# Last block's third w_in chunk loaded beside the fourth; a rank inside a second layer; the last routing steps reordered

## What is computed

```python
# 1. attention, 2 batches x 8 heads x 576 tokens x 64, keeping the 32 largest scores of a row
scores = q @ k.T / sqrt(64);  attn = softmax(scores where scores >= 32nd largest of the row)
x = (attn @ v)                         # -> 1152 tokens x 512
# 2. dense layer pair with a parametric relu
h = x @ w_in;  g = max(h, 0) + alpha * min(h, 0);  x2 = g @ w_out    # 512 -> 2048 -> 512
# 3. mixture of 8 experts, each token to its best 2
noisy = x2 @ w_gate + log1p(exp(x2 @ w_noise)) * noise
top2 of noisy per token; weights = softmax over those two
out[token] += weight * (relu(x2 @ w1[e]) @ w2[e])     # 512 -> 1024 -> 512
```

## Time and profile before

| what | value |
|---|---|
| median of 3 runs | 728.12 us (727.68 to 728.68) |
| the profiled execution | 731.02 us, of which the span of its instructions is 729.3 us |
| TensorE busy (matmul) | 663.6 us, 91% of the span |
| VectorE (DVE) busy | 528.5 us, 72% |
| ScalarE (ACT) busy | 466.8 us, 64% |
| GpSimd (POOL) busy | 392.9 us, 54% |
| attention of the last block ends | about 424 us |
| first expert item starts on TensorE | 477.08 us |

### The profile page before, as it was taken

One profiled execution on the slowest core, in us unless ns is written; L12 is line 12 of the kernel. 1 busy time (PEld: TensorE's weight loads), 2 busy tenths in 40 slices (PEclk: granted clock), 3 DMA queues, 4 the chain that ended last, 5 costly groups with the idle time before them and its releaser, 6 DMA issues.

```text
span 729.3 us, 13745 instructions
## 1 busy us (share of the span) xinstructions
PE 663.6 (91%) x4688; PEld 563.9 (77%) x4688; DVE 528.5 (72%) x1112; ACT 466.8 (64%) x881; POOL 392.9 (54%) x436
## 2 busy tenths in 40 slices
PE   2467789999989999999999999899999999999993
PEld 2346667887867888888888777688998999989993
DVE  5999999989769989898998352695565555555520
ACT  5788876787887787787777645755354553544511
POOL 3598898788787777677767766220220311302112
PEclk9987989999999999999999999999999999999997
DMA  9879436645418535264563769735935738457222
GB/s 284 357 257 386 153 153 226 237 161 184 189 20 282 184 132 213 92 245 161 194 212 116 276 236 353 240 118 192 291 100 205 223 103 279 122 181 238 72 32 36
DMA packets 39964, 141.01 MB, mean 193 GB/s; under 512 B 11152, under 2 KB 12176, under 8 KB 35856
## 3 DMA queue, kind: packets, MB, share of 16 engines
q1 hardware_dynamic: 35520, 130.25, 49.9%
q0 software_dynamic: 4384, 9.98, 6.3%
HBM read 113.70 MB, written 45.73 MB: 219 GB/s over the span
## 4 chain that ended last, share of the span: by engine, by line
PE 70%; POOL 13%; ACT 6%; issue 4%; DVE 4%; DMA 1%; SPq 0%; POOLq 0%; ACTq 0%; another core or an unknown queue 0%; DVEq 0%
PE bank L1261 11%; PE bank L1079 11%; PE ps_scores L1245 10%; PE bank L1042 7%; PE bank L1245 6%; PE bank L1018 6%; POOL expo L1763 4%; PE bank L1266 4%; PE bank L1047 3%; PE bank L1000 3%; PE ps_scores L969 3%; POOL w_in_parts L1775 2%; POOL k_parts L1720 2%; PE bank L1059 2%; PE bank L1280 1%
## 5 line engine op out<-in xcount | busy, mean ns | idle before, releaser
L441 DVE MAX8 top<-rest 128x8 f32<-128x576 f32 x216 | 152.4, 748 | 0.0
L1923 POOL DMA_INDIRECT out_dram<-ye,xe x24 | 42.8, 1785 | 190.0 <-ACT ye L1661 164.6
L1763 POOL TENSOR_TENSOR expo<-scores,expo 128x576 f32<-128x576 f32 x72 | 103.8, 1442 | 60.8 <-ACT scores L1354 60.6
L453 DVE MATCH_REPLACE8 rest<-top,rest 128x576 f32<-128x576 f32 x144 | 105.9, 744 | 0.0
L1079 PE MATMUL bank<-w_out_high,g_parts 128*128 128x512 f32 x288 | 99.7, 407 | 0.2 <-DVE g_parts L652 0.2
L659 DVE TENSOR_TENSOR w_lo<-raw,w_hi 128x1024 fp32r<-128x1024 f32 x64 | 78.0, 1225 | 19.4 <-ACT w_hi L1588 18.6
L1261 PE MATMUL bank<-w_hi,he_t 128*128 128x512 f32 x224 | 80.5, 400 | 0.0
L1018 PEld LDWEIGHTS bank<-v,prob_t 128*64 128x64 f32 (+1 forms) x1440 | 57.0, 144 | 29.5 <-ACT prob_t L1381 14.7
L1018 PE MATMUL bank<-v,prob_t 128*64 128x65 f32 (+1 forms) x1440 | 72.5, 240 | 5.2 <-ACT prob_t L1381 5.1
L1245 PE MATMUL ps_scores<-xe_t,w_hi 128*128 128x320 f32 x320 | 70.8, 308 | 0.0
L1588 ACT CAST w_hi<-raw 128x1024 fp32r<-128x1024 f32 x64 | 66.8, 1046 | 4.9 <-DMA raw<-w_dram 4.7
(11 more groups left out here) (232 smaller groups left out, 1625.4 us busy)
## 6 DMA issues: line engine op xcount, KB each, us to landing
raw<-w_dram SPq DMA_DIRECT2D x64, 512.0 KB, 11.6
w_in_parts<-w_parts_dram SPq DMA_DIRECT2D x15, 2048.0 KB, 7.9
x_sorted_dram<-x_sorted_dram SPq DMA_DIRECT2D x7, 2570.0 KB, 11.2
w_parts_dram<-w_in_parts SPq DMA_DIRECT2D x4, 2048.0 KB, 10.1
q_raw<-q_rows_dram SPq DMA_DIRECT2D x18, 256.0 KB, 4.7
w_in_raw<-w_in_dram SPq DMA_DIRECT2D x4, 1024.0 KB, 11.7
w_out_raw<-w_out_dram SPq DMA_DIRECT2D x4, 1024.0 KB, 14.3
xe<-x_sorted_dram SPq DMA_DIRECT2D x7, 514.0 KB, 4.4
```

The source lines that it names most:

```text
L441: nc.vector.max(dst, src).then_inc(chain if r < ROUNDS - 1 else dve_top, 1)
L453: nc.vector.match_replace(rest[:, k, :], top[:, (n + k) % 4, 8 * r:8 * r + 8], src, LOWEST).then_inc(chain, 1)
L1763: nc.gpsimd.tensor_tensor(expo[:, n % 4, :], scores[:, n % SBUFS, :], expo[:, n % 4, :], ALU.mult).then_inc(pool_prob, 1)
```

## The change

Seven edits.

1. `w_in_last` becomes two places, the first and second half of `w_lo0`. Chunk 2 of the last block is loaded into the first half, as soon as the last attention values are multiplied (`pe_pv`), behind chunk 3; before, it waited for `first_layer(8, 0)`. The first expert's w1 pieces, whose place this is, are loaded when `first_layer(8, 2)` is done; before, when chunk 2 had landed.
2. `second_layer(7, 2)` is cut in two: six matmuls before turn 0's rank and `first_layer(8, 0)`, six behind.
3. DVE scores block 7 (turn 1) ahead of `last_low_g(2)`; the picking stays behind `last_prelu(3)`.
4. ScalarE makes `high_weights(1)` behind `last_high_g(3)`; before, it stood ahead of `last_high_g(2)`.
5. With one block to pick for (turns 1 and 2), one comparison of 16 elements takes the place of two of 8.
6. Turn 2 reads the gates where TensorE leaves them (in the bank): ScalarE's copy of them (L1482) is gone, Abs and two DVE steps read the bank.
7. For block 8 the 0/1 matrix is made from the rank's bank directly, against row numbers that have the base taken off ahead of time (one new DVE step of 320 elements, `slots_ahead`, behind turn 1's placing); before, the place was added up first and compared then.

The diff, without the lines that only pass the new arguments:

```diff
-        w_in_last = w_lo0[:, 4 * PIECE:].rearrange("p (b n) -> p b n", b=2)
+        w_in_last = [w_lo0[:, n * 4 * PIECE:(n + 1) * 4 * PIECE].rearrange("p (b n) -> p b n", b=2) for n in range(2)]
...
+        slots_ahead = o_sb[:, :, :, :].rearrange("p a h d -> p (a h d)")[:, 0:GROUP]
...
-                for k in range(2):
+                if n == 1:
+                    step(v3.tensor_tensor(hot[:, :, :, a], iota_f[:, 0:EXPERTS].unsqueeze(1).to_broadcast([P, 2, EXPERTS]),
+                                          best_f[:, :, a:b].to_broadcast([P, 2, EXPERTS]), ALU.is_equal))
+                for k in range(2) if n > 1 else ():
...
             def place_last(b, turn, bank):
                 dve.wait_ge(pe_rank, turn + 1)
+                nc.vector.tensor_scalar(slot_hot[1], slots_ahead, bank[:, 0:1], picked[:, 0, b:b + 1], ALU.is_equal,
+                                        ALU.mult).then_inc(hot_slots, 1)
                 place_one(bank)
-                hot_slots_of(b, 1)
...
+                if c == 2:
+                    score_tokens(EARLY, EARLY + 1, 1)
                 last_low_g(c)
...
             last_prelu(3)
-            score_tokens(EARLY, EARLY + 1, 1)
             pick_experts(EARLY, EARLY + 1, 1)
...
             place_block(EARLY, 1, ps_pt4)
+            step(v3.tensor_scalar(slots_ahead, slots_row, base[:, 0:1], None, ALU.subtract))
...
-            score_tokens(BLOCKS - 1, BLOCKS, 2)
+            score_tokens(BLOCKS - 1, BLOCKS, 2, src=ps_h[:, 0:2 * EXPERTS])
...
-            sp.dma_start(w_in_last.rearrange("p b n -> p (b n)").bitcast(F32), w_parts[3]).then_inc(w_in_back[1], 16)
-            next_w_in(BLOCKS - 1, 2)
+            sp.dma_start(w_in_last[1].rearrange("p b n -> p (b n)").bitcast(F32), w_parts[3]).then_inc(w_in_back[1], 16)
             sp.wait_ge(pe_pv, HEADS * BLOCKS)
-            sp.wait_ge(w_in_back[0], 16 * (BLOCKS - 1))
+            sp.dma_start(w_in_last[0].rearrange("p b n -> p (b n)").bitcast(F32), w_parts[2]).then_inc(w_in_back[0], 16)
+            sp.wait_ge(pe_first, 4 * BLOCKS - 1)
             load_weights(0, 0, range(4))
...
-                w_in_c = w_in_last if alone and c == 3 else w_in_parts[:, c % 2]
+                w_in_c = w_in_last[c - 2] if alone and c >= 2 else w_in_parts[:, c % 2]
...
             x_transpose(j)
+            second_layer(j - 1, 2, range(2))
             pe.wait_ge(act_pt, HEADS * BLOCKS)
...
-            second_layer(j - 1, 2)
+            second_layer(j - 1, 2, range(2, 4))
...
-            high_weights(1, 0, 0)
             last_high_g(j, 2)
...
-            for c in range(2, 4):
+            for c in range(1, 4):
                 high_weights(c, 0, 0)
...
-            copy_gates(j, ps_h[:, 0:2 * EXPERTS])
-            softplus(j, j + 1, 2)
+            softplus(j, j + 1, 2, ps_h[:, EXPERTS:2 * EXPERTS])
```

More of the change, by code:

```diff
@@ L523, in _, with score_tokens @@
             v3 = nc.vector
-            def score_tokens(a, b, turn, sums=False):
+            def score_tokens(a, b, turn, sums=False, src=None):
                 dve.wait_ge(route_act, 4 * turn + 3)
-                step(v3.scalar_tensor_tensor(out=noisy[:, a:b, :], in0=gate[:, a:b, EXPERTS:], scalar=0.0,
+                if src is None:
+                    src = gate[:, a:b, :]
+                else:
+                    src = src.rearrange("p (b n) -> p b n", b=1)
+                step(v3.scalar_tensor_tensor(out=noisy[:, a:b, :], in0=src[:, :, EXPERTS:], scalar=0.0,
                                              in1=noisy[:, a:b, :], op0=ALU.max, op1=ALU.add))
                 step(v3.tensor_tensor(noisy[:, a:b, :], noisy[:, a:b, :], noise_sb[:, a:b, :], ALU.mult))
-                step(v3.tensor_tensor(noisy[:, a:b, :], noisy[:, a:b, :], gate[:, a:b, 0:EXPERTS], ALU.add))
+                step(v3.tensor_tensor(noisy[:, a:b, :], noisy[:, a:b, :], src[:, :, 0:EXPERTS], ALU.add))
                 for t in range(a, b):
@@ L1060, in h_transpose, with second_layer @@
                 mm.then_inc(pe_ht1, 1)
-            def second_layer(j, c):
+            def second_layer(j, c, ks=range(4)):
                 last = isinstance(j, int) and j == BLOCKS - 1
@@ L1075, in second_layer @@
                         wait(pe, act_x2t, j)
-                for k in range(4):
+                for k in ks:
                     at = slice((4 * chunk_of(j, c) + k) * MODEL, (4 * chunk_of(j, c) + k + 1) * MODEL)
@@ L1081, in second_layer @@
                                        stop=(c == CHUNKS - 1 and k == 3 and a == 1))
-                mm.then_inc(pe_second, 1)
+                if k == 3:
+                    mm.then_inc(pe_second, 1)
             def x2_transpose(j, dst=ps_y, src=x2_now, chunks=0):
@@ L1482, in copy_gates, with softplus @@
                 nc.scalar.copy(dst, src).then_inc(act_gate, 1)
-            def softplus(a, b, turn):
-                act.wait_ge(act_gate, b)
+            def softplus(a, b, turn, src=None):
                 part = noisy[:, a:b, :]
-                nc.scalar.activation(part, gate[:, a:b, EXPERTS:], ACT.Abs).then_inc(route_act, 1)
+                if src is None:
+                    act.wait_ge(act_gate, b)
+                    src = gate[:, a:b, EXPERTS:]
+                else:
+                    act.wait_ge(pe_gate, b)
+                    part = noisy[:, a, :]
+                nc.scalar.activation(part, src, ACT.Abs).then_inc(route_act, 1)
                 act.wait_ge(route_act, 4 * turn + 1)
```

## The result

| | kernel before | changed kernel |
|---|---|---|
| median, runs in turn on one chip | 728.89 us (726.92 to 731.22, 10 runs) | 724.26 us (723.23 to 726.49, 10 runs) |
| ratio of the two | | 0.9948, interval 0.9935 to 0.9962 |
| profiled execution, span | 731.02 us, 729.3 us | 723.99 us, 722.2 us |
| idle ahead of turn 0's rank | 1.71 us | 0.34 us |
| wait for chunk 2 of w_in | 1.21 us | none |

The change is faster by 0.52%, 3.8 us (2.8 to 4.7); forecast were 5.3 us. The direction is right and the size is not: the gain is 1.5 us smaller than forecast, more than the interval allows.

What follows compares the result with a forecast made beforehand. The prediction took TensorE alone to set the pace, so gains before the first expert item are kept. Terms -1.37 - 1.64 - 1.21 + 0.35 - 0.92 - 0.50 = -5.29 us took 728.12 to 722.8 us, range 721.3 to 725.0 us.

Steps and rivals of the forecast that it cites:

- the profiled execution's differences carry over to the median: Whole sum: savings worked out on the 731.02 us profiled execution were taken off the 728.12 us median.
- Turn 0's rank: Six matmuls fill TensorE's idle time ahead of this rank, cutting it from 1.71 to 0.34 us: -1.37 us.
- The clock: Behind turn 0's rank, less idle time keeps TensorE at full clock, so `first_layer(8, 0)` shortens: -1.64 us.
- rival (a): Clock falls all the same behind turn 0's rank, so 1.64 us stay: 724.5 us; chance 10%.
- Chunk 2's load: Ahead of `first_layer(8, 2)`: the load, given out earlier, arrives in time and TensorE's wait goes: -1.21 us.
- Piece 0: First expert weight piece, estimated to land 5.0 us after issue, makes ScalarE's cast 0.4 us late: +0.35 us.
- Turn 1's order: Reordered ScalarE and DVE steps remove waits ahead of `second_layer(8, 2)` (0.17 us) and turn 1's rank (0.75 us): -0.92 us.
- Turn 2: Chain from gates to placing loses the gate copy, a comparison and a sum; bank reads add nothing: -0.50 us.
- rival (b): Piece 0 lands 6.5 to 9 us after issue; TensorE stands ahead of `second_layer(8, 2)`: 724.3 to 726.6 us; chance 14%.
- Rival (d): Front gain given back at late chunk 2, early rows or first item's weights: 727.5 us; chance 4%.
- Rival (e): Clock also stays up behind turn 2's rank, up to 1 us more gain: 721.8 us; chance 15%.

Runs made afterwards that it cites:

- A: First chip: kernel before unchanged 728.48 us (0.9998); parts of the change were run here separately.
- C: Third chip, both kernels unchanged: kernel before 728.77 us (1.0003), changed kernel 724.70 us (0.9952).
- D: Fourth chip, both kernels unchanged: kernel before 729.00 us (1.0001), changed kernel 723.88 us (0.9926).
- edit 1 alone: Kernel before plus only chunk 2's load in its new place and the expert's pieces loaded behind `first_layer(8, 2)`: 727.56 us, 0.9986.
- edits 3 to 7 alone: Changed kernel with chunk 2's load, the pieces and `second_layer(7, 2)` as before: 726.47 us (0.9966) on the first chip, 726.78 us (0.9975) on the third.
- edit 2 undone: Changed kernel with all of `second_layer(7, 2)` behind `first_layer(8, 0)` again, on the second chip: 731.38 us, 1.0021 of the kernel before.
- B: Second chip: changed kernel run again, unchanged, 730.07 us (1.0012 of the kernel before); three variants of the changed kernel followed.
- E: Fifth chip: changed kernel unchanged, 731.19 us (1.0040 of the kernel before); with later piece 0 cast and extra matmuls, 729.12 us (1.0028).
- edit 2 alone: Kernel before plus only six matmuls of `second_layer(7, 2)` moved ahead of turn 0's rank: 728.19 us, 0.9993.
- second profile of the change: Changed kernel run again without alteration, on the second chip: 730.07 us, 1.0012 of the kernel before.
- pieces later: Changed kernel with the first four weight pieces given out behind `first_layer(8, 3)` instead of `first_layer(8, 2)`, on the second chip: 733.64 us, 1.0058 of the kernel before.

## Why the prediction was right in direction and wrong in size

The forecast said that the profiled execution's differences carry over to the median. That is the step that failed. The profiled execution of before was 2.9 us above the median, and part of that excess lay in the very waits that were to be removed. Four profiles of the kernel before (the first, and those of chips A, C and D) give, to the item, 49.47, 47.12, 48.79 and 46.68 us, mean 48.02; three of the change where it is faster (the first, C, D) 44.44, 44.22 and 44.01, mean 44.22. The difference is 3.8 us, against 5.03 us between the first two alone. Cut at the starts of TensorE's rows, it adds up as follows (us; minus is faster).

| stretch of TensorE's timeline | forecast | first two profiles | mean of four before, three after |
|---|---|---|---|
| six matmuls that left the stretch behind the rank | -1.37 | -1.37 | -1.37 |
| `first_layer(8, 0)`: the clock | -1.64 | -1.59 | -0.79 |
| second chunk to the end of `first_layer(8, 2)`: chunk 2's load | -1.21 | -1.52 | -1.15 |
| wait ahead of `second_layer(8, 2)`: piece 0 | +0.35 - 0.17 | +0.87 | +0.71 |
| from there through turn 1's rank | -0.75 | -1.20 | -0.80 |
| turn 2 up to block 8's rows | -0.50 | -0.50 | -0.50 |
| block 8's rows to the first item | 0 | +0.28 | +0.10 |
| sum | -5.29 | -5.03 | -3.80 |

Two terms were mis-sized, the clock by 0.85 us and piece 0 by 0.53 us; together they are 1.4 of the 1.5 us that are missing. By terms:

- **Turn 0's rank**: -1.37 us, right in every profile (0.34 to 0.36 us idle).
- **The clock**: the term that failed most. The forecast counted -1.64 us in full and weighed only whether the clock would fall in the changed kernel; it never asked whether it falls in every execution of the kernel before. In the four profiles of that kernel `first_layer(8, 0)` takes 4.43, 2.84, 4.42 and 2.85 us, so the fall is worth 1.59 us in two of them and nothing in the other two: -0.79 us on the mean. Over all kernels with 1.71 us idle at this place it fell in five profiles of eight (the first one, edit 1 alone, edits 3 to 7 alone on A, the kernel before on C, edit 2 undone) and not in three (the kernel before on A and D, edits 3 to 7 on C). With 0.34 to 0.36 us the clock behind the rank was 1.00 in all twelve profiles, so rival (a) did not happen.
- **Chunk 2's load**: -1.21 us counted. The wait did go; but in the four profiles it is 1.21, 0.85, 1.07 and 0.25 us, mean 0.85 us. Against that, a stop costs some 0.3 us more than its bracket, which the forecast left out. That the term comes out near is luck: the two errors cancel.
- **Piece 0**: +0.18 us counted on the wait ahead of `second_layer(8, 2)` (+0.35, less the 0.17 us that turn 1's order was to remove), +0.71 us measured (waits of 1.04, 0.91, 0.69 us, mean 0.88, where the kernel before has 0.15 to 0.19). The mechanism was right; the load took 5.4 us, not the estimated 5.0. The Trainium skill, page "DMA: Bandwidth & Descriptors", section "Anatomy of one DMA", gave the prediction an estimate of 3.2 us and no wait. The section gives that fit for DMAs issued by GpSimd, and these loads are issued by SyncE; the 5.4 us measured here are far from it.
- **Turn 1's order**: -0.75 us counted for the rank. In the other three profiles its wait is 0.21, 0.22 and 0.22 us, mean of the four 0.35. In the first profile ScalarE had stood 0.43 us for TensorE ahead of a relu of `last_relu_both(3)`, which the one on chip A has without a bracket. Here too a stop costs more than its bracket: 0.17 us ahead of the rank, and the rank itself takes 463.36 - 462.72 = 0.64 us behind a wait and 456.89 - 456.53 = 0.36 without one. So -0.80 us, near the forecast by luck again.
- **Turn 2**: -0.50 us counted and measured, 0.30 ahead of the rank and 0.20 behind it. A bank as source cost nothing, as taken. The Trainium skill, page "VectorE: DVE Perf Modes", section "The TRN2 errata", would have the two steps 0.13 us longer, by the prediction's estimate; 0.17 us before and after says no.

That the mean of so few profiles meets the measured 3.8 us so closely is luck in part: on C the two profiles differ by 4.6 us where the times say 3.5 (2.1 to 5.0), on D by 2.7 where the times say 5.4 (3.5 to 7.4). The single terms rest on the traces; the times can't tell them apart.

Stops of rival (b)'s size happened on B and E, but not by the landing of piece 0: ScalarE has no wait for it there, other than where it was given out later. Rival (d)'s place, the early rows, showed only when piece 0's cast was moved. Rival (e) did not happen: the clock fell behind turn 2's rank in every profile of the change, and it took matmuls put there to hold it.

That the profiles' spans differ by 7.1 us is chance in part: block 8's first transpose stands at 427.61 us before and at 425.93 after, 1.7 us apart ahead of anything that the change touches, and in the other profiles of the kernel before at 424.95 to 427.32.

## What to carry to other kernels

Before a wait of one profiled execution goes into a sum, compare that execution with the median, and take a second profile of the same kernel: waits for loads, for the clock, and short waits between engines differed by up to 1.6 us from one execution to the next here, and the execution that was above the median had more of what was to be removed. Look for the next late load behind whatever is gained: edit 2 alone gave its 1.4 us back there. Follow a transfer that is issued later to the engine that takes it in order: what stands behind it there waits too. And where a gain is half a per cent, measure it on more than one chip: this one was there on two and in the first measurement, and gone on two others.

## What the hardware showed that was not expected

**The chip matters.** The kernel before takes about the same on all five chips (728.2 to 729.0 us). The change is at 0.9926 to 0.9952 on two and in the first measurement, and at 1.0012 and 1.0040 on B and E. There its S is 55.71 and 57.43 us, against 50.5 to 50.9. All kernels that were profiled on B and E have edit 1, and in their traces ScalarE gets TensorE's results later than TensorE's rows have them: 3.2 us for `first_layer(8, 2)` in the row of the kernel with edit 2 undone, and 6.8 us for `first_layer(8, 3)` in the second profile of the change (444.57 against 451.42 us). In both, ScalarE sees nothing late until about 16 us behind block 8's first transpose, which is the end of `first_layer(8, 2)` in one and its start in the other, and in two kernels (edit 2 undone, pieces later) results are late before any piece is given out. The second profile of the change and the one with piece 0's cast moved, with and without that cast in between, reach the same copy (`last_copy_h1(3)`) 26.3 and 26.2 us behind that transpose: it isn't ScalarE's own work that is late. The kernel before is not slow in time on these chips, but there is no profile of it on one, and of kernels without edit 1 no other was run there; so whether edit 1 is what exposes the delay wasn't tried. The cause stays open; that TensorE really ran slower there than its rows say is what the other engines' rows suggest, not shown.

**The clock is not a function of the program.** The same stretch of instructions with the same 1.71 us of idle time got 2.4 GHz in one execution and 1.2 GHz in another: the kernel before on A and on C, edits 3 to 7 alone on C and on A. The chip doesn't decide it either, since both happened on A and both on C, in kernels with the same TensorE instructions up to there.

**A stop can cost more than the idle time listed.** From the second chunk to the end of `first_layer(8, 2)` it is 0.3 us more than the bracket in all four profiles of the kernel before, at turn 1's rank 0.17 us ahead of it and 0.28 us in it. Part of it is how rows are drawn: matmuls of 512 columns that follow one another are 0.40 us long and start 0.23 us apart, and a bracket counts only from the end of the last row. Turn 0's rank has no such cost: it takes 0.44 us behind 1.71 us of idle time and behind 0.34 us.
